# Rows normalised by ScalarE instead of VectorE in a fused attention, Fourier mixing and MLP kernel

## What is computed

```python
# second block: x is (4, 576, 512), the attention output with heads side by side
X = np.fft.fft(x, axis=1)
X = np.fft.fft(X, axis=2)
u = x + np.real(X).astype(np.float32)
mu = np.mean(u, axis=-1, keepdims=True)
var = np.mean((u - mu) ** 2, axis=-1, keepdims=True)
un = (u - mu) / np.sqrt(var + 1e-06)
u2 = u + np.maximum(un @ w_ch1, 0.0) @ w_ch2
# third block
gate = 1.0 / (1.0 + np.exp(-gate_pre))   # gate_pre: five taps of a causal convolution over u2
out = gate * (u2 @ w_val) @ w_out
```

## Time and profile before

| | us |
|---|---|
| median of 3 runs | 814.59 (813.22 to 815.72) |
| the profiled execution | 811.06 |
| its span | 809.2 |
| TensorE matmul busy | 737.7 (91%) |
| VectorE busy | 403.7 (50%) |
| ScalarE busy | 191.8 (24%) |
| GpSimd busy | 148.8 (18%) |
| mean granted clock of TensorE | 0.979 |

### The profile page before, as it was taken

One profiled execution on the slowest core, in us unless ns is written; L12 is line 12 of the kernel. 1 busy time (PEld: TensorE's weight loads), 2 busy tenths in 40 slices (PEclk: granted clock), 3 DMA queues, 4 the chain that ended last, 5 costly groups with the idle time before them and its releaser, 6 DMA issues.

```text
span 809.2 us, 15617 instructions
## 1 busy us (share of the span) xinstructions
PE 737.7 (91%) x5960; PEld 546.8 (68%) x5960; DVE 403.7 (50%) x927; ACT 191.8 (24%) x417; POOL 148.8 (18%) x126
## 2 busy tenths in 40 slices
PE   1779755989999998999999998999999999999998
PEld 1555343777776776777776776787776777777776
DVE  3437276743653684643643684743643780113552
ACT  1336431222221212222221223222212122111101
POOL 7105569980100210000100210000100300000000
PEclk9999956999999999999999999999999999999999
DMA  9875046213100004513101105413100000000001
GB/s 292 239 171 175 25 137 156 49 29 77 28 1 31 31 30 138 98 29 75 30 1 31 31 29 151 85 29 79 25 2 1 1 29 30 2 1 1 2 15 45
DMA packets 42106, 49.15 MB, mean 61 GB/s; under 512 B 4784, under 2 KB 35568, under 8 KB 40944
## 3 DMA queue, kind: packets, MB, share of 16 engines
q1 hardware_dynamic: 33392, 31.69, 16.4%
q10 hardware_dynamic: 8640, 16.43, 5.9%
HBM read 43.38 MB, written 4.72 MB: 59 GB/s over the span
## 4 chain that ended last, share of the span: by engine, by line
PE 68%; POOL 10%; DVE 7%; SPq 5%; issue 4%; DMA 3%; ACT 1%; ACTq 0%; DVEq 0%; POOLq 0%
PE P L539 20%; PE Y L556 20%; PE P L668 4%; PE Y L657 4%; PE A L565 3%; PE Y L668 3%; SPq L416 3%; POOL w L1322 3%; POOL w L1326 2%; PE A L526 2%; PE A L519 2%; PE A L618 1%; SPq L408 1%; PE A L607 1%; PE A L462 1%
## 5 line engine op out<-in xcount | busy, mean ns | idle before, releaser
L539 PE MATMUL P<-unT,w_wv 128*128 128x288 f16 x1536 | 213.3, 290 | 10.3 <-DVE hT L1095 5.0
L556 PE MATMUL Y<-hT,w 128*128 128x288 f16 x1536 | 215.0, 286 | 3.9 <-POOL w L1328 2.4
L1095 DVE SCALAR_TENSOR_TENSOR hT<-P,hT 128x288 f16<-128x288 f32 x128 | 58.4, 457 | 263.0 <-ACT hT L779 263.0
L539 PEld LDWEIGHTS P<-unT,w_wv 128*128 128x128 f16 x1536 | 149.7, 99 | 55.7 <-issue 12.0
L556 PEld LDWEIGHTS Y<-hT,w 128*128 128x128 f16 x1536 | 144.8, 98 | 48.3 <-issue 9.6
L779 ACT ACTIVATE hT<-P 128x288 f16<-128x288 f32 x128 | 52.6, 411 | 198.9 <-PE P L539 198.8
L1131 DVE SCALAR_TENSOR_TENSOR gate<-xT,cw,gate 128x288 f32<-128x288 f32 x128 | 66.4, 519 | 4.5
L750 ACT ACTIVATE prob_or_un<-prob_or_un 73x288 f32<-73x288 f32 (+1 forms) x52 | 23.3, 448 | 128.7 <-DVE prob_or_un L968 128.7
L1261 POOL MEMSET x<- 1x512 f32 x4 | 2.1, 516 | 228.5 <-ACT x L768 228.5
L565 PE MATMUL A<-sdft,pair_or_folded 128*128 128x289 f32 (+5 forms) x102 | 32.8, 444 | 4.6 <-DVE pair_or_folded L1025 4.6
L297 POOL TENSOR_TENSOR x<-x,fb 128x256 f32<-128x256 f32 (+1 forms) x12 | 11.8, 987 | 116.7 <-DVE fb L1036 116.7
(11 more groups left out here) (169 smaller groups left out, 894.2 us busy)
## 6 DMA issues: line engine op xcount, KB each, us to landing
kl<-qk_win SPq DMA_DIRECT2D x38, 140.0 KB, 4.2
ql<-qk_win SPq DMA_DIRECT2D x19, 256.0 KB, 3.8
vl<-v_win SPq DMA_DIRECT2D x72, 65.0 KB
pair_or_folded<-qk_pool SPq DMA_DIRECT2D x8, 580.0 KB, 5.7
pair_or_spectrum<-qk_pool SPq DMA_DIRECT2D x8, 580.0 KB, 7.1
out<-ot ACTq DMA_DIRECT2D x32, 144.0 KB, 1.8
w_wv<-w_ch ACTq DMA_DIRECT2D x4, 1024.0 KB, 11.9
w<-w_ch ACTq DMA_DIRECT2D x4, 1024.0 KB, 6.6
```

Of the source, the lines that this page charges most:

```text
L539: last = mm(P[s % 2][:, 0:HN], w1s(k, f, wt), unT[:, ut, k, ha * HN:(ha + 1) * HN], start=k == 0 and wt + ut == 0, stop=k == KD - 1 and wt ...
L556: last = mm(Y[d][:, 0:HN], w2s(f, d, wt), hT[s % 3][:, ht, :], start=f == 0 and wt + ht == 0, stop=f == KF - 1 and wt == 1)
L1095: nc.vector.scalar_tensor_tensor(out=hT[s % 3][:, 1, :], in0=P[s % 2][:, 0:HN], scalar=0.0, in1=hT[s % 3][:, 0, :], op0=ALU.max, op1=ALU.s ...
```

## The change

VectorE's `normalise`, a `tensor_scalar` that subtracts the mean and multiplies by `rstd`, goes. ScalarE gets a `normalise` of the same name that computes x * rstd + shift with one `activation` for each tile. `shift` is minus mean times `rstd`; `inv_std` on GpSimd makes it with two more small instructions, of 128 x 2 elements, in its code before and after the power. ScalarE waits for `shift_done`.

```diff
@@ -127,6 +127,7 @@
         stats = sb("stats", [128, 6, 6])
         mv = sb("mv", [128, 3, 2, 2])
         rstd = sb("rstd", [128, 3, 2])
+        shift = sb("shift", [128, 3, 2])
         un = [prob_or_un[:, DM * i:DM * (i + 1)] for i in range(2)] + [p[:] for p in probT]
 
         xT = sb("xT", [128, KD, TAPS - 1 + N])
@@ -212,6 +213,8 @@
         bn_done = sem("bn_done")
         var_eps = sem("var_eps")
         rstd_done = sem("rstd_done")
+        mean_down = sem("mean_down")
+        shift_done = sem("shift_done")
         un_done = sem("un_done")
         uT_ps = sem("uT_ps")
         unT_ps = sem("unT_ps")
@@ -814,6 +817,17 @@
             def un_columns(b, i):
                 act.wait_ge(unT_ps, 6 * b + i + 1)
                 columns(column_banks(b, i)[1], unT[:, 0], i).then_inc(unT_hi, 1)
+
+            def normalise(b, j):
+                act.wait_ge(shift_done, 3 * b + j + 1)
+                for h in range(2):
+                    r = XROWS[j + 3 * h]
+                    if j == 0 and h == 0:
+                        act.wait_ge(transposed, NU * (b + 1))
+                    if j == 2:
+                        act.wait_ge(unT_ps, 6 * b + h + 1)
+                    nc.scalar.activation(un[(2 * j + h) % 4][0:r, :], x[0:r, j + 3 * h, :], ACT.Identity, bias=shift[0:r, j, h:h + 1],
+                                         scale=rstd[0:r, j, h:h + 1]).then_inc(un_done, 1)
 
             def load_weights(c):
 
@@ -909,13 +923,20 @@
                     load_weights(2 * KD + 1)
                     for i in range(6):
                         u_columns(b, i, m)
+                        if i % 2 == 0:
+                            normalise(b, i // 2)
                         un_columns(b, i)
                 else:
                     if b is not None:
-                        for i in range(4):
-                            un_columns(b, i)
+                        normalise(b, 0)
+                        un_columns(b, 0)
+                        un_columns(b, 1)
+                        normalise(b, 1)
+                        un_columns(b, 2)
+                        un_columns(b, 3)
                     outputs(m, 0)
                     if b is not None:
+                        normalise(b, 2)
                         un_columns(b, 4)
                         un_columns(b, 5)
                     gate_e(m, 1)
@@ -1050,15 +1071,6 @@
                     dve.sem_inc(passed, 1)
                     i = nc.vector.bn_aggr(mv[0:r, j, h, :], stats[0:r, j + 3 * h, :])
                 i.then_inc(bn_done, 1)
-
-            def normalise(b, j):
-                dve.wait_ge(rstd_done, 3 * b + j + 1)
-                for h in range(2):
-                    r = XROWS[j + 3 * h]
-                    if j == 2:
-                        dve.wait_ge(unT_ps, 6 * b + h + 1)
-                    nc.vector.tensor_scalar(un[(2 * j + h) % 4][0:r, :], x[0:r, j + 3 * h, :], mv[0:r, j, h, 0:1],
-                                            rstd[0:r, j, h:h + 1], ALU.subtract, ALU.mult).then_inc(un_done, 1)
 
             def weight_scale(i):
 
@@ -1190,14 +1202,11 @@
                     weight_scale(1)
                     statistics(b, 0)
                     combine(b, 1)
-                    normalise(b, 0)
                     statistics(b, 1)
                     combine(b, 2)
-                    normalise(b, 1)
                     columns(b, 0)
                     statistics(b, 2)
                     columns(b, 1)
-                    normalise(b, 2)
                     for i in range(2, 6):
                         columns(b, i)
                 elif b is None:
@@ -1286,7 +1292,13 @@
                 pool.sem_inc(passed, 1)
                 nc.gpsimd.tensor_scalar(rstd[0:r, j, :], mv[0:r, j, :, 1], 1e-6, None, ALU.add).then_inc(var_eps, 1)
                 pool.wait_ge(var_eps, 3 * b + j + 1)
+                pool.sem_inc(passed, 1)
+                nc.gpsimd.tensor_scalar(shift[0:r, j, :], mv[0:r, j, :, 0], -1.0, None, ALU.mult).then_inc(mean_down, 1)
                 pt(rstd[0:r, j, :], rstd[0:r, j, :], mhalf[0:r, :], ALU.pow).then_inc(rstd_done, 1)
+                pool.wait_ge(mean_down, 3 * b + j + 1)
+                pool.wait_ge(rstd_done, 3 * b + j + 1)
+                pool.sem_inc(passed, 1)
+                pt(shift[0:r, j, :], shift[0:r, j, :], rstd[0:r, j, :], ALU.mult).then_inc(shift_done, 1)
 
             def step(b, first=False):
                 zero_rows(b, first)
```

## The result

The changed kernel took 820.64 us (median, 819.37 to 822.48, 4 runs) beside 815.11 of the kernel before on the same chip: ratio 1.0080 [1.0051, 1.0109]. It is slower by 5.5 us by the two medians and by about 6.5 by the ratio, where the prediction had 2.4. The profiled execution took 819.37 us, its span is 817.5 (809.2 before), its mean clock 0.969 (0.979 before).

The account below looks back on a forecast made before the run. TensorE's work was taken as 68% of the chain of waits. 811.06 + 1.2 (pairs) - 0.5 (chunks) + 1.6 (clock) = 813.4, with the median 3.5 above: 816.9, said as 817.0; range 813.5 to 821.0.

Parts of the forecast that it names:

- the rival with falls of the clock: Clock falls at the loop steps' new waits too, one to three falls at 1.6: 818.6 to 821.8; chance 20%.
- Second pair: Second pair of transposes, each loop step: no wait left for VectorE, projection starts earlier, -1.9 us.
- Third pair: Third pair of transposes, each loop step: TensorE waits for ScalarE, which normalises behind the fourth store, +2.3 us.
- The waits of 2.0 us ahead of the third pair: TensorE's waits ahead of the third pair in the loop steps: no clock fall counted, taken as none.
- GpSimd's chunks: First step, once: mix_rev -1.1 us, added instructions +0.5 and 0.1, so weight chunks start earlier, -0.5 us.
- The clock at the eighth chunk: First step, once: TensorE's wait for the eighth weight chunk grows to 4.2 us, clock likely falls, +1.6 us.
- The sum: Whole kernel: 811.06 + 1.2 - 0.5 + 1.6 = 813.4; the runs' median 3.5 above, so 816.9, said as 817.0.
- The two terms of the first step: First step: GpSimd's weight chunks, -0.5 us, and the clock fall at the eighth chunk, +1.6 us.
- `mix_rev`'s 1.92: GpSimd, first step: 1.92 us beside VectorE's normalisation, 0.83 without; removing that neighbour gives -1.1 us.

Follow-up runs that it names:

- e5_filled4: Changed kernel plus four matmuls with unused results ahead of the third pair of transposes in each loop step, filling TensorE's wait: 814.00 us, ratio 1.0005.
- e8: Kernel before with only the loop steps changed, ScalarE normalising the third pair after the second of four outputs: 807.77 us, ratio 0.9931.
- e9: The kernel before, unchanged, measured and profiled once more: 813.50 us, ratio 1.0005.
- e11: Changed kernel with the first step as in the kernel before, so only the loop steps are changed: 819.29 us, ratio 1.0088.
- e12_gpsimd_only: Kernel before plus GpSimd's negation and product for each pair and a wait for the product, result unused; VectorE still normalises: 811.05 us, ratio 0.9978.
- e4_first_only: Changed kernel with ScalarE normalising in the first step alone; loop as in the kernel before, GpSimd's list included: 814.77 us, ratio 1.0021.

## Why the prediction was wrong

The direction was right and the time, 820.64 us, lies in the range, which reached to 821.0 for the sake of the rival with falls of the clock. The size was not: +6.5 us by the ratio against +2.4. By its own steps:

- *Second pair, -1.9 us a step*: right. 9.51 us from the first block of `val` to the projection, after 11.39; no wait left. With an activation at 0.81 and the shift ready at 285.7 instead of 283.85 + 1.75 (the first pair's transposes stand 1.75 us later in this profile), the margin was a tenth or two thinner than forecast, and enough.
- *Third pair, +2.3 us a step*: right in mechanism and size, 10.96 us for a forecast 10.98, released by ScalarE, 2.01 and 0.30 us in brackets.
- *"The waits of 2.0 us ahead of the third pair are of the size at which it once held (2.13, 2.40) and once fell (2.46); I take none."* This is the step that failed: the term was put at nothing. The clock fell in 8 of 9 such places and cost 1.69 us each, 5.1 where it falls in all three steps. e5_filled4 shows that it is the idling: same arrival of the data, no idling, and the loss is gone. Two waits that had held, against one that had fallen, were no reason to take nothing; the 28 at the turn of a step, 15 of them with a fall, would have put it at about half of the price. Why it is 8 of 9 here is open. This wait stands ahead of a short pair of transposes (0.40 us each) with another 0.30 between them, which fits, but no run changed these alone. That rival was written down, at 20% and 1.6 a fall; with all three it gave 821.8, and the runs gave 820.6.
- *GpSimd's chunks, -0.5 us*: wrong sign, +0.54 from the first `mix_rev` to the first chunk. `mix_rev` came back at 0.83 as forecast. But a pair costs 0.9 us more, not 0.5: the starts alone were counted, not the 0.20 and 0.17 us in which GpSimd waits for its own result. And the first two pairs' share was not absorbed. That the first chunk still starts at 121.10, as forecast (121.15), is luck: the first `mix_rev` starts 1.08 us earlier in this execution.
- *The clock at the eighth chunk, +1.6*: the fall is there after 4.70 us of waiting, as I had it (4.2), and costs 2.3 us there. But it is there in e8, e9 and e11 as well, whose first step is the old one. The term was mostly a difference between executions and not of the change; the forecast had added it to the one profile in which the clock had held. Without it the forecast would have been +0.7.
- *The sum*: 3 x 0.4 for the pairs and 3 x 1.69 for the clock are 6.3 us, and 6.5 was measured. The two terms of the first step, +1.1 together in the forecast, are not needed for it.

A step that the prediction left out altogether: why VectorE's normalisation of the second pair took 2.00 us. It put `mix_rev`'s 1.92 down to the neighbour on VectorE and did not ask the same of VectorE's 2.00 beside `mix_rev`. e12_gpsimd_only shows the two apart.

## What to carry to other kernels

A new wait of TensorE has two prices, its length and the clock behind it, and the second can be the larger part: here 1.7 us a fall against a net 0.4. A wait of this length that held once in a trace doesn't show that it holds: other steps and other profiles ended waits of the same size the other way, so give the fall its share in the sum. Before moving an operation to a less busy engine, look at where it lands in that engine's list: the same two activations cost 4.1 us in a step behind the fourth store and nothing behind the second. And an operation that takes twice its usual time beside another engine's may need only that the other starts a little later, here 0.8 us behind it.

## What the runs showed of the hardware

- The clock fell after 2.01 + 0.30 us of idling around short transposes (8 of 9) and after 1.04 + 0.30 (2 of 3). It did not fall at the second pair of the kernel before and of e4_first_only, after 1.26 to 1.29 us between 4 us of matmuls and 1.2 of transposes (9 places), nor in e5_filled4 with 0.30 alone (3). At the turn of a loop step it held after 13 waits of 1.99 to 2.93 us and fell after 15 of 2.07 to 3.08: the two overlap, and no length in these profiles divides them. The same wait doesn't always end the same way (e11's middle step).
- A whole fall costs 1.7 us, the same in a group of f32 matmuls (9.72 - 8.03) and in one of f16 (4.78 - 3.11). At the eighth chunk, over three groups, it was 1.7 (e9_before_again) and 2.3 (the changed kernel).
- GpSimd waits 0.17 to 0.23 us for its own result where its next instruction is made to wait for it. The same product of 128x2 took 0.20 us in the changed kernel, where ScalarE has the tiles next, and 0.47 in e12 beside VectorE's normalisation.
- The Trainium skill (SBUF — State Buffer, SBUF: two separate sides) says that GpSimd and a VectorE instruction in a two-port mode lock a shared pair of ports against each other. The rows agree from VectorE's side, 1.00 us for two tiles in e12 and 2.00 beside `mix_rev`; no row here shows in which mode VectorE's instruction runs.
